# Attention loop written out group by group: three sets of load buffers, attention outputs three groups behind, x stored from SyncE's queue

## The chip, the cores and the metric

The kernel runs on one core of one Trainium2 chip. The metric is the device time of one execution in microseconds (us), lower is better. The core has five engines that work side by side: TensorE (PE: matrix products, its weight loads are listed as PEld), VectorE (DVE), ScalarE (ACT), GpSimd (POOL) and SyncE (SP, which here only issues transfers). DMA transfers are issued from SP's queue, ACT's queue or POOL's queue and are moved by 16 DMA engines that all of them share.

## The reference

Attention over 32 learned memory slots, then a dense layer with a gate, then a mixture of eight experts:

```python
a = exp(phi - max(phi, axis=2)); a = a / (sum(a, axis=2) + 1e-9)      # 8 x 8 heads, 576 x 32
k_m, v_m = a^T k, a^T v                                               # 32 x 64 per head
s = q k_m^T / 8; attn = exp(s - max(s)); attn = attn / (sum + 1e-9)   # 576 x 32 per head
x = attn v_m                            # all heads: 4608 tokens x 512
h = x @ w_in                            # 4608 x 2048
x2 = (h * sigmoid(1.702 * h)) @ w_out   # 4608 x 512
e = argmax(x2 @ w_gate)                 # one of 8 experts for each token
out = gate * sigmoid(x2 @ w_output_gate)[e] * (relu(x2 @ w1[e]) @ w2[e])
```

## The kernel before

The program has three stages. Stage A is the attention, in 16 groups of four heads (NG = 16; batch b is groups 2b and 2b+1). Stage B is the dense layer and the routing, in nine tiles of 512 tokens. Stage C is the experts, in blocks of 128 tokens. The change touches stage A and the first tile of stage B.

**A group of stage A.** SP loads `phi` (288 KB), `k` and `v` in one piece `kvm` (1152 KB) and `q` (576 KB) into one of two sets of buffers. DVE takes the maximum of phi (`phi_in`, L1147), ACT the exponential (L880), PE transposes it (L627, L630), ACT copies it out (`a_out`, L890), PE forms k_m and v_m (L647, L652), ACT scales them (`kv_scale`, L899), POOL lays v out in blocks (`v_blocks`, L1571), PE transposes k (L662), ACT copies it (`k_out`, L906), and PE makes the scores (L675). DVE transposes the scores and subtracts their maximum (`less_max`, L1158 to L1162), ACT takes the exponential (`exp_scores`, L884), DVE forms the inverse sums (`inverses`, L1169 to L1175), POOL multiplies (`normalize`, L1563), DVE transposes the result into `pT` (`attn_out`, L1181), PE multiplies it with v in two halves (`out_half`, L619), and ACT copies each half (`x_out`, L915) into `keep`, where x stays in on-chip memory (`xo` for the last batch).

**The order of the work** is written by hand. Each engine runs one program, and what it does for group g is mixed with work for the groups behind: in PE's `group(g)` stand the k/v products of g, the transposes of phi of g+1, the k transposes of g, the first half of the output of g-2, the scores of g, and the second half of the output of g-2. DVE's `group(g)` is `phi_in(g+1)`, `inverses(g)`, `less_max(g-1)`, `attn_out(g-2)`. There is one `pT`, which DVE fills and PE reads. Groups 0 to 2 and the last ones are written out, the others are a hardware loop of four groups a pass (`groups`, L376).

**SP's queue.** SP issues transfers in program order, and each waits until the buffer is free: `load_phi(g)` for exp of g-2 (L440), the k/v load for the k/v product of g-2, the q load for the scores of g-2. Between them it loads four quarters of `w_in` into the two halves of `raw`, which POOL splits into a high and a low part (`split_w_in`, L1548 and L1550; `split_w`, L1538 and L1540, for `w_out`). Each `load_w(n)` waits until part n-2 has been split.

**Into stage B.** ACT makes the high part of tile 0's x (`first_x_hi`, L941) in group 15, all four pieces. After group 15 it issues the store of batches 0 to 5 to DRAM from its own queue (`store_kept`, L921; 2 x 3456 KB), then batch 6 (2 x 576 KB), and later batch 7 (`store_last`, L927; 1152 KB). Tiles 1 and on load their x back from there. PE starts stage B with `mm1(0, 0)` (L702, 12 products of 128x512), `mm1(0, 1)` and `mm1(0, 2)` with the outputs of groups 14 and 15 between them; then `mm2(0, 0)`, `mm2(0, 1)` (L734), `mm1(0, 3)`, `mm2(0, 2)`, `mm1(0, 4)` and so on. `mm1(0, 4)` needs 12 split parts of weights, `mm2(0, f)` needs 5 + 2f: four parts are split in stage A, so for `mm1(0, 4)` POOL has to split parts 4 to 11 after it.

Of the kernel before, what the change touches and what calls it, by code (L numbers as in the profile page):

```python
# [91 lines left out]
def build(nc, q, kv, phi, w_in, w_out, gates, w1, w2, cst, out):  # L92
# [11 lines left out]
    with ExitStack() as ctx:  # L104
# [32 lines left out]
        with ExitStack() as a:  # L137


            vbd = sbt(a, "vbd", [P, 4, 2 * D])  # L140
            sc = [sbt(a, f"sc{u}", [P, S]) for u in range(2)]
            scs = sbt(a, "scs", [P, 2, 3, SB + 2])
            sbt(a, "before_xs", [P, K1 * T - 2 * S - 6 * (SB + 2)])

            qT, kvm, phT = [], [], []
            for u in range(2):
                qT.append(sbt(a, f"qT{u}", [P, QA // 2, HG, M]))
                kvm.append(sbt(a, f"kvm{u}", [P, QA * D * 2]))
# [8 lines left out]
            sbt(a, "before_aT", [P, S])  # L157
            aT = sbt(a, "aT", [P, S])
            am = sbt(a, "am", [P, S])
            sbt(a, "before_kmT", [P, QA * D])  # L160
            kmT = sbt(a, "kmT", [P, P])
            mask = sbt(a, "mask", [P, 2 * D])
            kvs = sbt(a, "kvs", [P, 2 * D])
            sbt(a, "before_pT", [P, S])
            pT = sbt(a, "pT", [P, S])
            xo = sbt(a, "xo", [P, 2, 2, S])
# [67 lines left out]
        s_phi = [sem(f"phi_loaded{u}") for u in range(2)]  # L234
        s_q = [sem(f"q_loaded{u}") for u in range(2)]
        s_kvl = [sem(f"kv_loaded{u}") for u in range(2)]
# [87 lines left out]

        def kept_at(b, u):

            return KEEP + u * KEPT * S + b * S
# [5 lines left out]
        def kept_stored(eng):  # L333

            eng.wait_ge(s_xfirst, 16 * 2)
            eng.wait_ge(s_xkept, 16 * 2)

        stage = [xo[:, 0, 0, 0:P], xo[:, 0, 0, P:2 * P]]
# [36 lines left out]

        def groups(eng, body):  # L376

            for g in range(3):
                body(g, g // 2, g)
            with eng.Fori(0, (NG - 4) // 4) as m:  # L380
                for j in range(4):
                    body(4 * m + (3 + j), 2 * m + (3 + j) // 2, (3 + j) % 4)
            body(NG - 1, B - 1, 3)
# [49 lines left out]
        def _(sp):  # L433
# [5 lines left out]
            def load_phi(g, b, u):  # L439

                wait(sp, s_aT, g - 1)
                sp.dma_start(phT[u][:], phi[bass.ds(g * P, P), :]).then_inc(s_phi[u], 16)

            def load_qkv(g, b, u):
# [5 lines left out]
                sp.dma_start(qT[u][:].rearrange("p c h n -> p (c h n)"), q[bass.ds(g * P, P), :]).then_inc(s_q[u], 16)  # L450
# [10 lines left out]
            load_phi(0, 0, 0)  # L461
# [3 lines left out]
            load_qkv(0, 0, 0)  # L465
            load_phi(1, 0, 1)
            load_qkv(1, 0, 1)
            def sp_group(g, b, r):

                u = r % 2  # L470
                if not isinstance(g, int) or g + 2 < NG:
                    load_phi(g + 2, b + 1, u)
                    load_qkv(g + 2, b + 1, u)

                if isinstance(g, int) and 1 <= g < 3:
                    load_w(g - 1, w_in_part(g - 1, 0))
                if isinstance(g, int) and g >= NG - 5 and g < NG - 3:
                    load_w(g - (NG - 5) + 2, w_in_part(g - (NG - 5) + 2, 0))


            for g in range(3):
                sp_group(g, g // 2, g)
            with sp.Fori(0, (NG - 8) // 4) as m:
                for j in range(4):
                    sp_group(4 * m + (3 + j), 2 * m + (3 + j) // 2, (3 + j) % 4)
            for g in range(NG - 5, NG - 2):
                sp_group(g, g // 2, g % 4)

# [18 lines left out]
            def sp_tile(t, first=False, last=False):  # L507
# [3 lines left out]
                if first:  # L511
                    for k in range(1, 4):
# [5 lines left out]
                        if k == 1:  # L518
                            sp.wait_ge(s_xfirst, 16 * 2)
                            sp.wait_ge(s_pT, NG)  # L520
                            load_x(t + 1)
# [81 lines left out]
        def _(pe):  # L603
            def out_half(g, r, i, bank=None):
# [3 lines left out]
                if i == 0:  # L608
                    wait(pe, s_pT, g + 1)
                    wait(pe, s_vbd, g + 1)  # L610


                if isinstance(g, int) and g >= NG - 2:
                    pe.wait_ge(s_xo, 2 * (NG - 2) + (1 if g == NG - 1 else 0))
                else:
                    wait(pe, s_xo, 2 * g - 1 + i)
                for pair in range(2):
                    rows = slice(pair * 64, pair * 64 + 64)
                    mm = pe.matmul(ps[:, bank + pair, 0:HS], vbd[rows, r, :], pT[rows, i * HS:(i + 1) * HS],  # L619
# [14 lines left out]
            def group(g, b, r):  # L634

                u = r % 2
                has_out = not isinstance(g, int) or g >= 2
                last = isinstance(g, int) and g == NG - 1

                wait(pe, s_kvl[u], 16 * (b + 1))  # L640
                if not isinstance(g, int) or g >= 3:
                    wait(pe, s_xo, 2 * g - 5)
                hold(pe, s_am, g + 1)
# [12 lines left out]
                if not last:  # L656
# [3 lines left out]
                hold(pe, s_kk, g + 1)  # L660
# [5 lines left out]
                if has_out:  # L666
                    out_half(g - 2, (r + 2) % 4, 0)

                wait(pe, s_kmT, g + 1)
                wait(pe, s_q[u], 16 * (b + 1))  # L670
                hold(pe, s_dv, DVE_A * g)
# [7 lines left out]
                if has_out:  # L679
                    out_half(g - 2, (r + 2) % 4, 1)  # L680

            wait(pe, s_cst, 2 * 16)
            a_transposes(0)
            groups(pe, group)
# [22 lines left out]

            mm1(0, 0)
            for i in range(2):
                out_half(NG - 2, (NG - 2) % 4, i, (4, 2)[i])  # L710
            mm1(0, 1)
            for i in range(2):
                out_half(NG - 1, (NG - 1) % 4, i, (6, 4)[i])
# [160 lines left out]
        def _(act):  # L874
            def exp_phi(g, u):
# [4 lines left out]
                act.activation(aT[:], phT[u][:], ACT.Exp, bias=amax[:, u, 0:1], accum_out=scs[:, u, 1, SB:SB + 1]).then_inc(s_aT, 1)  # L880
# [27 lines left out]
            def x_out(g, b, u, i, bank=None):  # L908
                bank = (4, 2)[i] if bank is None else bank
                hold(act, s_o, 2 * g + i + 1)  # L910
                if isinstance(b, int) and b == KEPT:
                    to = xo[:, u, :, i * HS:(i + 1) * HS]
                else:
                    to = keep_v[:, :, bass.ds(kept_at(b, u) + i * HS, HS)]
                act.copy(to, ps[:, bank:bank + 2, 0:HS]).then_inc(s_xo, 1)  # L915

            def store_kept(b, n, stored):

                act.wait_ge(s_xo, 4 * (b + n))
                for u in range(2):  # L920
                    act.dma_start(xT_dram[2 * u * P:(2 * u + 2) * P, b * S:(b + n) * S].rearrange("(a p) n -> p a n", a=2),  # L921
                                  keep_v[:, :, kept_at(b, u):kept_at(b + n, u)]).then_inc(stored, 16)
# [14 lines left out]
            def first_x_hi(c):  # L937

                act.wait_ge(s_sc, NG - 1)
# [3 lines left out]
            def group(g, b, r):  # L943
                u = r % 2
                last = isinstance(g, int) and g == NG - 1
                if not last:
                    exp_phi(g + 1, 1 - u)
                if not isinstance(g, int) or g >= 3:
                    x_out(g - 3, b - 2 + u, 1 - u, 1)
# [4 lines left out]
                if not isinstance(g, int) or g:  # L954
                    exp_scores(g - 1, 1 - u)
                k_out(g)
                if not last:
                    a_out(g + 1)
                else:
                    store_kept(0, KEPT - 1, s_xfirst)  # L960
                if not isinstance(g, int) or g >= 2:
                    x_out(g - 2, b - 1, u, 0)
# [118 lines left out]
            x_out(NG - 1, B - 1, 1, 0, 6)  # L1081
            x_out(NG - 1, B - 1, 1, 1, 4)
# [60 lines left out]
        def _(dve):  # L1143
            def phi_in(g, b, u):
                wait(dve, s_phi[u], 16 * (b + 1))

                dve.tensor_reduce(amax[:, u, 0:1], phT[u][:], AX.X, ALU.max, negate=True).then_inc(s_amax, 1)  # L1147
# [29 lines left out]
            def attn_out(g, u):  # L1177
# [11 lines left out]
            def group(g, b, r):  # L1189
# [536 lines left out]
```

## Time and profile before

| | |
|---|---|
| median of 3 runs | 1368.81 us (1366.98 to 1371.24) |
| profiled execution, its own time | 1368.63 us |
| its span in the trace | 1367.0 us |
| granted TensorE clock, mean | 0.987 of full speed |
| PE busy | 1317.9 us (96%), 6866 instructions |
| DVE busy | 635.1 us (46%) |
| ACT busy | 390.8 us (29%) |
| POOL busy | 549.2 us (40%) |
| chain that ended last | PE 85%, DMA 3% of the span |

The chain is followed back from the last instruction: at each step to what released it. Busy time is an average over the stages, so a change in one stage is read from that stage's part of the trace. "PEclk" is the clock that was granted to TensorE as a share of full speed (2.4 GHz; 0.50 is 1.2 GHz). "DMA share" is the mean busy share of the 16 DMA engines.

### The profile page before, as it was taken

Reading aid. Unit: us, or ns where it says so; the run is one execution under the profiler, and the core shown is the slowest. Engines: PE = TensorE matmul, PEld = TensorE weight load, DVE = VectorE, ACT = ScalarE, POOL = GpSimd, SP = SyncE. Lnnn points to the kernel's source line nnn. Section 1 sums busy time; section 2 is a strip of 40 time slices with the busy share of each in tenths; the row PEclk is TensorE's granted clock in tenths of the full one; section 3 lists DMA queues with packets and bytes.
Section 4 is the critical chain, followed back from the end, with each engine's and each line's share of the span. In section 5 each row is a group of like instructions: output and inputs, shape, how many; then the busy total and the mean of one; then the engine's idle time right before and its main releaser. Section 6 shows DMA issues by size and latency. Waiting matters only on the chain.

```text
span 1367.0 us, 23811 instructions
## 1 busy us (share of the span) xinstructions
PE 1317.9 (96%) x6866; PEld 1056.9 (77%) x6867; DVE 635.1 (46%) x1291; ACT 390.8 (29%) x725; POOL 549.2 (40%) x648
## 2 busy tenths in 40 slices
PE   5888899999999999999999999999999999999997
PEld 3445688888888888888888888887788888888886
DVE  4776243353343433534334344346655555555553
ACT  3564122222222222322222222223332222232221
POOL 2335683353454433443444334511533343433332
PEclk9899999999999999999999999999999999999999
DMA  8897437556566465465654646547884789648882
GB/s 316 319 352 304 156 130 210 192 184 183 189 213 179 169 192 190 151 189 177 180 187 163 192 172 173 177 159 261 228 229 101 202 228 268 177 118 254 251 245 63
DMA packets 152376, 274.19 MB, mean 201 GB/s; under 512 B 16916, under 2 KB 54053, under 8 KB 149765
## 3 DMA queue, kind: packets, MB, share of 16 engines
q1 hardware_dynamic: 94468, 196.04, 43.2%
q10 hardware_dynamic: 44672, 45.63, 13.2%
q0 software_dynamic: 13184, 31.88, 7.5%
q8 instruction: 27, 0.44, 0.1%
q14 instruction: 25, 0.20, 0.0%
HBM read 144.98 MB, written 100.45 MB: 180 GB/s over the span
## 4 chain that ended last, share of the span: by engine, by line
PE 85%; DMA 3%; POOL 1%; issue 1%; DVE 1%; ACT 0%; ACTq 0%; POOLq 0%
PE ps L702 28%; PE ps L734 28%; PE ps L804 14%; PE ps L775 14%; DMA raw<-in_moe_w_in 2%; PE ps L744 1%; DMA cq<-ch 1%; DMA cmeta<-record_scratch 0%; POOL W L1550 0%; ACTq L1036 0%; DVE chT L1371 0%; POOL W L1548 0%; DVE cqT L1358 0%; POOL out L1663 0%; POOL W L1540 0%
## 5 line engine op out<-in xcount | busy, mean ns | idle before, releaser
L702 PE MATMUL ps<-xs,W 128*128 (+1 forms) x1728 | 419.2, 391 | 3.0 <-POOL W L1550 3.0
L734 PE MATMUL ps<-W,gs 128*128 128x512 f32 x1728 | 417.0, 390 | 4.3 <-POOL W L1540 4.2
L734 PEld LDWEIGHTS ps<-W,gs 128*128 128x128 f32 x1728 | 325.2, 188 | 73.1 <-issue 5.0
L702 PEld LDWEIGHTS ps<-xs,W 128*128 128x128 f32 x1728 | 324.0, 188 | 73.3 <-issue 6.5
L1234 DVE TENSOR_TENSOR gate<-ps,gate 128x512 f32<-128x512 f32 x144 | 99.6, 692 | 373.0 <-ACT gate L978 370.4
L978 ACT ACTIVATE gate<-ps 128x512 f32<-128x512 f32 x144 | 86.2, 598 | 477.6 <-PE ps L702 453.4
L804 PE MATMUL ps<-W,chT 128*128 (+1 forms) x936 | 218.4, 389 | 2.5 <-DVE chT L1371 2.5
L775 PE MATMUL ps<-W,cx 128*128 (+1 forms) x936 | 218.6, 389 | 0.8 <-issue 0.8
L1604 POOL CAST whi<-raw 128x512 fp32r<-128x512 f32 x128 | 82.9, 648 | 331.4 <-DMA raw<-in_moe_w 331.4
L804 PEld LDWEIGHTS ps<-W,chT 128*128 128x128 f32 x936 | 175.5, 188 | 39.9 <-issue 3.6
L775 PEld LDWEIGHTS ps<-W,cx 128*128 128x128 f32 x936 | 175.5, 188 | 37.8 <-issue 1.4
L1606 POOL TENSOR_TENSOR raw<-raw,whi 128x512 f32<-128x512 f32 x128 | 171.5, 1340 | 21.5 <-POOL whi L1604 19.1
L1236 DVE TENSOR_TENSOR gs<-gate,gs 128x512 fp32r<-128x512 f32 x144 | 118.5, 823 | 99.9 <-ACT gs L982 99.2
L364 POOL DMA_DIRECT2D crec<-record_scratch x160 | 90.4, 565 | 184.5 <-DMA out<-cy,cmeta 120.2
L982 ACT CAST gs<-gate 128x512 fp32r<-128x512 f32 x144 | 89.4, 621 | 112.1 <-DVE gate L1234 109.5
L1043 ACT CAST chT<-cqT 128x512 fp32r<-128x512 f32 x41 | 25.4, 621 | 202.6 <-issue 159.8
L1663 POOL DMA_INDIRECT out<-cy,cmeta x39 | 44.1, 1132 | 78.4 <-ACT cy L1051 71.0
L1612 POOL DMA_INDIRECT record_scratch<-rec,posi x36 | 36.2, 1006 | 90.4 <-DVE posi L1300 81.8
L1371 DVE TENSOR_TENSOR chT<-cqT,chT 128x512 fp32r<-128x512 f32 x78 | 53.2, 691 | 39.2 <-ACT chT L1043 37.6
L1335 DVE TENSOR_TENSOR cx<-cxT,cx 128x512 fp32r<-128x512 f32 x40 | 43.7, 1091 | 56.7 <-ACT cx L1011 54.3
L1349 DVE TENSOR_SCALAR ch<-ps 128x512 f32<-128x512 f32 x37 | 25.5, 690 | 68.6 <-PE ps L775 68.3
L1358 DVE STREAM_TRANSPOSE cqT<-cq 128x512 f32<-128x512 f32 x78 | 50.6, 687 | 13.3 <-DMA cq<-ch 10.7
(163 smaller groups left out, 786.1 us busy)
## 6 DMA issues: line engine op xcount, KB each, us to landing
W<-expert_scratch SPq DMA_DIRECT2D x24, 2048.0 KB, 11.2
raw<-in_moe_w SPq DMA_DIRECT2D x128, 256.0 KB, 2.8
expert_scratch<-whi SPq DMA_DIRECT2D x128, 256.0 KB, 2.6
expert_scratch<-raw SPq DMA_DIRECT2D x128, 256.0 KB, 2.9
cq<-ch ACTq DMA_DIRECT2D x156, 128.0 KB
kvm<-in_kv SPq DMA_DIRECT2D x16, 1152.0 KB, 7.3
crec<-record_scratch POOLq DMA_DIRECT2D x160, 64.0 KB
qT<-in_q SPq DMA_DIRECT2D x16, 576.0 KB, 5.1
```

The costliest lines, as they stand in the source:

```text
L364: eng.dma_start(crec[b * M:(b + 1) * M, r % 3], rows[:, b * P:(b + 1) * P].rearrange("(h n) d -> n h d", n=M)).then_inc(loaded, 16)
L702: mm = pe.matmul(ps[:, f % 2, :], W[:, col:col + P], xs[:, bass.ds(x0 + (x_lo * K1 + c) * T, T)], start=(c == 0 and w_lo + x_lo == 0), sto ...
L734: mm = pe.matmul(ps[:, 2 + s, :], gs[:, f % 2, g_lo, s * P:(s + 1) * P], w_out_sb[:, f, w_lo, :], start=(f == 0 and g_lo + w_lo == 0), sto ...
L775: mm = pe.matmul(ps[:, 3 * u + j, :], cx[:, u, x_lo, c, :], W[:, bass.ds(col, 512)], start=(c == 0 and x_lo + w_lo == 0), stop=(c == K1 - ...
L804: mm = pe.matmul(ps[:, 5 + r % 2, :], chT[:, r % 2, h_lo, c, :], W[:, bass.ds(col, DM)], start=(c == 0 and h_lo + w_lo == 0), stop=(c == C ...
L978: act.activation(gate[:, f % 2, :], ps[:, f % 2, :], ACT.Sigmoid, scale=QTOK).then_inc(b_sig, 1)
L982: act.copy(gs[:, f % 2, 0, :], gate[:, f % 2, :]).then_inc(b_ghi, 1)
L1234: dve.tensor_tensor(gate[:, f % 2, :], ps[:, f % 2, :], gate[:, f % 2, :], ALU.mult).then_inc(b_g, 1)
L1236: dve.tensor_tensor(gs[:, f % 2, 1, :], gate[:, f % 2, :], gs[:, f % 2, 0, :].bitcast(F32), ALU.subtract).then_inc(b_glo, 1)
L1371: dve.tensor_tensor(by_h(1, j), cqT[:, j * 512:(j + 1) * 512].rearrange("p (h c n) -> p h c n", h=2, n=M), by_h(0, j).bitcast(F32), ALU.su ...
L1604: pool.tensor_copy(whi[:, u, :], raw[:, u, :]).then_inc(e_hi, 1)
L1606: pool.tensor_tensor(raw[:, u, :], raw[:, u, :], whi[:, u, :].bitcast(F32), ALU.subtract).then_inc(e_lo, 1)
```

## The change

1. **Load buffers.** There are three sets in place of two (`qT2`, `kvm2`, `phT2` are new), taken in turn by g % 3. `load_phi(g)`, `load_kv(g)` and `load_q(g)` wait for exp, k/v product and scores of group g-3 in place of g-2.
2. **Outputs.** `out_half` for group g-3 stands where that of g-2 stood, and there are two `pT`, taken in turn. `x_out` follows one group later. More of the outputs therefore falls behind group 15: a pair of halves is now ahead of, and one behind, `mm1(0, 0)`.
3. **Unrolled.** `groups` is gone; all 16 groups are written out on every engine.
4. **Weights.** The four quarters of `w_in` are loaded and split at groups 5, 6, 9, 10 in place of 1, 2, 11, 12 on SP (2, 3, 12, 13 on POOL).
5. **x of tile 0.** `first_x_hi` is made two pieces in group 14 and two in group 15.
6. **Stores.** Batches 0 to 4 are stored in one go (2 x 2880 KB), 5 and 6 one by one, and from SP's queue, in program order ahead of `load_w(6)`. Batch 7 stays on ACT's queue.

Core of the diff:

```diff
-        s_phi = [sem(f"phi_loaded{u}") for u in range(2)]
+        s_phi = [sem(f"phi_loaded{u}") for u in range(3)]
...
+        FIRST = 5
+        QUARTER = (5, 6, 9, 10)
...
-            def load_phi(g, b, u):
-                wait(sp, s_aT, g - 1)
+            def load_phi(g):
+                wait(sp, s_aT, g - 2)
...
-                wait(sp, s_kv, g - 1)
-                sp.dma_start(kvm[u][:], kv[bass.ds(g * P, P), :]).then_inc(s_kvl[u], 16)
-                wait(sp, s_sc, g - 1)
+            def load_kv(g):
+                wait(sp, s_kv, g - 2)
+                sp.dma_start(kvm[g % 3][:], kv[g * P:(g + 1) * P, :]).then_inc(s_kvl[g % 3], 16)
+            def load_q(g):
+                wait(sp, s_sc, g - 2)
...
+            for g in range(1, NG):
+                load_phi(g)
+                load_kv(g)
+                load_q(g)
+                if g in QUARTER:
+                    c = QUARTER.index(g)
+                    load_w(c, w_in_part(c, 0))
             load_w(K1, w_out_v[0])
             load_w(K1 + 1, w_in_part(0, 1))
+            store_kept(0, FIRST, s_xfirst)
+            for b in range(FIRST, KEPT):
+                store_kept(b, 1, s_xkept)
...
-                if has_out:
-                    out_half(g - 2, (r + 2) % 4, 0)
+                if g >= 3:
+                    out_half(g - 3, 0)
...
+            out_half(NG - 3, 0)
             mm1(0, 0)
-            for i in range(2):
-                out_half(NG - 2, (NG - 2) % 4, i, (4, 2)[i])
+            out_half(NG - 3, 1)
+            out_half(NG - 2, 0)
             mm1(0, 1)
+            out_half(NG - 2, 1)
             for i in range(2):
-                out_half(NG - 1, (NG - 1) % 4, i, (6, 4)[i])
+                out_half(NG - 1, i, (6, 4)[i])
             mm1(0, 2)
...
-                if last:
-                    for c in range(K1):
-                        first_x_hi(c)
+                if g >= NG - 2:
+                    for c in range(2):
+                        first_x_hi(2 * (g - (NG - 2)) + c)
...
-                wait(dve, s_o, 2 * g)
-                dve.transpose(pT[:], sc[u][:]).then_inc(s_pT, 1)
+                wait(dve, s_o, 2 * (g - 1))
+                dve.transpose(pT[g % 2][:], sc[g % 2][:]).then_inc(s_pT, 1)
```

How it moves two pieces of the program. First SP, from the loads of group 15 to the first parts of weights of stage B (`raw` holds a part of weights, `xT_scratch` is x in DRAM). Before:

```order
L442 DMA phT<-in_phi 128x576
L447 DMA kvm<-in_kv 128x2304
L450 DMA qT<-in_q 128x1152
L455 DMA raw<-in_moe_w_out 128x512
L455 DMA raw<-in_moe_w_in 128x512
L455 DMA raw<-in_moe_w_out 128x512
L455 DMA raw<-in_moe_w_in 128x512
```

and with the change:

```order
L442 DMA phT<-in_phi 128x576
L447 DMA kvm<-in_kv 128x2304
L452 DMA qT<-in_q 128x1152
L464 DMA raw<-in_moe_w_out 128x512
L464 DMA raw<-in_moe_w_in 128x512
L458 DMA xT_scratch<-keep 128x2x2880 x2
L458 DMA xT_scratch<-keep 128x2x576 x4
L464 DMA raw<-in_moe_w_out 128x512
L464 DMA raw<-in_moe_w_in 128x512
```

The six stores now stand between parts 4 and 5 and parts 6 and 7.

Second PE, from the k/v products of group 15 to `mm2(0, 0)` (`pT` with `vbd` is an output, `xs` with `W` is `mm1`, `W` with `gs` is `mm2`). Before:

```order
L647 MATMUL ps<-kvm,am 32x128 x16
L652 MATMUL ps<-kvm,am 32x128 x4
L662 MATMUL ps<-ident,kvs 64x128 x2
L619 MATMUL ps<-pT,vbd 128x288 x2
L675 MATMUL ps<-qT,kmT 32x288 x8
L619 MATMUL ps<-pT,vbd 128x288 x2
L702 MATMUL ps<-xs,W 128x512 x12
L619 MATMUL ps<-pT,vbd 128x288 x4
L702 MATMUL ps<-xs,W 128x512 x12
L619 MATMUL ps<-pT,vbd 128x288 x4
L702 MATMUL ps<-xs,W 128x512 x12
L734 MATMUL ps<-W,gs 128x512 x24
```

and with the change:

```order
L643 MATMUL ps<-kvm,am 32x128 x16
L648 MATMUL ps<-kvm,am 32x128 x4
L658 MATMUL ps<-ident,kvs 64x128 x2
L618 MATMUL ps<-pT,vbd 128x288 x2
L671 MATMUL ps<-qT,kmT 32x288 x8
L618 MATMUL ps<-pT,vbd 128x288 x4
L699 MATMUL ps<-xs,W 128x512 x12
L618 MATMUL ps<-pT,vbd 128x288 x4
L699 MATMUL ps<-xs,W 128x512 x12
L618 MATMUL ps<-pT,vbd 128x288 x6
L699 MATMUL ps<-xs,W 128x512 x12
L733 MATMUL ps<-W,gs 128x512 x24
```

Two output halves more (four products) stand behind group 15's own work: one ahead of `mm1(0, 0)` and one ahead of `mm1(0, 2)`, and the outputs beside group 15's scores belong to group 12 in place of 13.

## Rows read from the trace of the kernel before

**Rows 1.** Chain that ended last, first 200 us: start us, us, what.

```profile
121.78 12.74 DMA raw<-in_moe_w_in
...
148.64 4.34 PE ps L702 x12
152.97 2.72 PE ps L734 x12
```

**Rows 2.** Windows: us, busy us (instructions) per engine, granted clock, DMA share, GB/s.

```profile
12.00:18.00 6.00, 3.08 (x32) 1.65 (x36) 0.98 (x3) 1.59 (x5) 0.45 (x1) 1.00 1.02 425
20.00:104.00 84.00, 69.41 (x992) 36.30 (x988) 60.56 (x113) 46.76 (x100) 28.37 (x33) 0.88 0.93 336
69.00:69.50 0.50, 0.50 (x7) 0.12 (x5) 0.19 (x1) 0.50 (x2) 0.00 (x0) 1.00 0.82 166
70.00:70.50 0.50, 0.50 (x12) 0.30 (x4) 0.50 (x2) 0.50 (x2) 0.00 (x0) 1.00 0.98 406
76.71:82.20 5.49, 4.67 (x79) 2.57 (x77) 4.50 (x9) 3.70 (x9) 2.13 (x2) 1.00 0.98 342
106.00:114.00 8.00, 4.17 (x71) 2.28 (x72) 7.11 (x13) 5.82 (x12) 4.35 (x5) 1.00 0.05 18
115.00:140.00 25.00, 21.85 (x108) 15.26 (x92) 11.32 (x17) 8.85 (x14) 11.33 (x13) 0.95 1.00 409
```

**Rows 3.** Waits, 0 to 120 us: us in total, times, longest us.

```profile
DVE csum L1147 <- DMA phT<-in_phi: 27.7, 16, 3.7
...
PE ps L619 <- DVE pT L1181: 15.2, 10, 2.1
```

**Rows 4.** DVE in order of time: start us, us, what [idle before <-releaser].

```profile
18.34 0.75 DVE L1147 TENSOR_REDUCE csum<-phT 128x1 f32<-128x576 f32 x1 [3.70 <-DMA phT<-in_phi]
...
23.98 0.75 DVE L1147 TENSOR_REDUCE csum<-phT 128x1 f32<-128x576 f32 x1 [2.30 <-DMA phT<-in_phi]
...
75.06 0.75 DVE L1147 TENSOR_REDUCE csum<-phT 128x1 f32<-128x576 f32 x1 [0.49 <-DMA phT<-in_phi]
...
80.93 0.75 DVE L1147 TENSOR_REDUCE csum<-phT 128x1 f32<-128x576 f32 x1 [0.88 <-DMA phT<-in_phi]
...
102.89 0.75 DVE L1147 TENSOR_REDUCE csum<-phT 128x1 f32<-128x576 f32 x1 [3.24 <-DMA phT<-in_phi]
```

**Rows 5.** PE in order of time, 20 to 165 us.

```profile
28.93 1.33 PE L619 MATMUL ps<-pT,vbd 64*128 64x288 f32 x4 [1.96 <-DVE pT L1181]
...
81.51 0.76 PE L619 MATMUL ps<-pT,vbd 64*128 64x288 f32 x4
...
117.02 3.20 PE L702 MATMUL ps<-xs,W 128*128 128x512 f32 x12
...
148.64 4.34 PE L702 MATMUL ps<-xs,W 128*128 128x512 f32 x12 [2.99 <-POOL W L1550]
```

**Rows 6.** SP, ACT and POOL in order of time, seven places.

```profile
67.84 0.33 SPq L447 DMA_DIRECT2D kvm<-in_kv  x1
...
110.69 2.18 ACT L941 CAST xs<-keep 128x512 fp32r<-128x512 f32 x4
...
113.76 0.98 ACTq L921 DMA_DIRECT2D xT_scratch<-keep  x2
...
119.87 0.33 SPq L455 DMA_DIRECT2D raw<-in_moe_w_out  x1
...
130.62 0.61 POOL L1538 CAST W<-raw 128x512 fp32r<-128x512 f32 x1 [8.86 <-DMA raw<-in_moe_w_out]
...
156.42 0.61 POOL L1538 CAST W<-raw 128x512 fp32r<-128x512 f32 x1 [0.86 <-DMA raw<-in_moe_w_out]
...
161.13 0.61 POOL L1538 CAST W<-raw 128x512 fp32r<-128x512 f32 x1 [0.81 <-DMA raw<-in_moe_w_out]
```

**Rows 7.** DMA issues, 0 to 130 us: KB each, median us to landing.

```profile
kvm<-in_kv SPq DMA_DIRECT2D x16, 1152.0 KB, 7.3
...
phT<-in_phi SPq DMA_DIRECT2D x16, 288.0 KB, 5.2
```

More of the change, by code:

```diff
@@ L374, in wait_records @@
                 wait(eng, c_rec[r], 80 * (i // RING if r == EARLY else i // RING + 1))
[L376 to L383, printed above, removed]
         def tiles(eng, tile):
@@ L603, in _, with out_half @@
         def _(pe):
-            def out_half(g, r, i, bank=None):
+            def out_half(g, i, bank=None):
                 bank = (4, 2)[i] if bank is None else bank
                 if i == 0:
[L609 to L614, printed above, removed]
+                    pe.wait_ge(s_pT, g + 1)
+                    pe.wait_ge(s_vbd, g + 1)
+                if g == NG - 1:
+                    pe.wait_ge(s_xo, 2 * (NG - 2) + 1 + i)
                 else:
@@ L632, in a_transposes, with group @@
                 tr.then_inc(s_atr, 1)
[L634 to L643, printed above, removed]
+            def group(g):
+                u = g % 3
+                pe.wait_ge(s_kvl[u], 16 * (g // 3 + 1))
+                wait(pe, s_xo, 2 * (g - 4) + 1)
+                pe.wait_ge(s_am, g + 1)
                 out_of = lambda h: ps[h * M:(h + 1) * M, 4, 3 * P:4 * P].rearrange("p (w d) -> p w d", w=2)
@@ L654, in group @@
                 mm.then_inc(s_kv, 1)
-                if not last:
+                if g + 1 < NG:
                     a_transposes(g + 1)
                 wait(pe, s_kmT, g)
-                hold(pe, s_kk, g + 1)
+                pe.wait_ge(s_kk, g + 1)
                 for i in range(2):
@@ L677, in group @@
                 mm.then_inc(s_sc, 1)
-                if has_out:
-                    out_half(g - 2, (r + 2) % 4, 1)
-            wait(pe, s_cst, 2 * 16)
+                if g >= 3:
+                    out_half(g - 3, 1)
+            pe.wait_ge(s_cst, 2 * 16)
             a_transposes(0)
-            groups(pe, group)
+            for g in range(NG):
+                group(g)
             def mm1(t, f):
@@ L1187, in x_lo, with group @@
                                   ALU.subtract).then_inc(b_xlo, 1)
-            def group(g, b, r):
-                u = r % 2
-                last = isinstance(g, int) and g == NG - 1
-                two = not isinstance(g, int) or g >= 2
-                if not last:
-                    phi_in(g + 1, b + u, 1 - u)
-                inverses(g, u, two, True)
-                if not isinstance(g, int) or g:
+            def group(g):
+                u = g % 2
+                if g + 1 < NG:
+                    phi_in(g + 1)
+                inverses(g, u, g >= 2, True)
+                if g:
                     less_max(g - 1, 1 - u)
-                if two:
-                    attn_out(g - 2, u)
+                if g >= 2:
+                    attn_out(g - 2)
             dve.memset(padrec[:], 0.0).then_inc(b_setup, 1)
@@ L1216, in _ @@
             dve.wait_ge(s_cst, 2 * 16)
-            groups(dve, group)
+            for g in range(NG):
+                group(g)
             dve.wait_ge(b_xhi, K1)
```

171 lines of the change are left out of this document (78 added, 93 removed).

## The prediction

> **What bounds the kernel now.** I read the page's chain first: PE is 85% of it, and DMA, its second part, lies in its first 150 us. [Rows 1] show where: the chain waits 12.74 us for one 256 KB part of weights at 121.78 us and reaches `mm1(0, 4)` on PE at 148.64; from there on it is PE without a break. So whatever brings `mm1(0, 4)` forward shortens the kernel by as much, and nothing else in this change does. I then split the 148.64 us into three stretches. G14 is the instant at which DVE takes the maximum of phi of group 15 (102.89 us, [rows 4]); T is the start of `mm1(0, 0)` (117.02 us, [rows 5]); the third ends at `mm1(0, 4)`.
>
> *First stretch.* DVE waited 27.7 us in all 16 groups for phi to land ([rows 3]), and phi is what it begins a group with. Between two such waits a group takes it 80.93 - 0.88 - 75.06 = 4.99 us ([rows 4]), while the groups came (102.89 - 23.98) / 12 = 6.58 us apart. PE's own work in a group is 4.67 us at full clock ([rows 2], fifth line). So loads set the pace. But not by bandwidth alone: in 20 to 104 us the DMA engines are busy 0.93 of the time and yet move 336 GB/s, while in 12 to 18 us, when SP had issued several loads ahead, they moved 425 GB/s at full share ([rows 2]). The difference stands at the start of a load that was issued late: SP issues k/v at 67.84 us ([rows 6]), and the share stays at 0.82 while only 166 GB/s move at 69.0 to 69.5; a microsecond later it is 406 ([rows 2]). With two sets of buffers each group has such starts.
>
> *Second stretch.* 14.1 us from G14 to T. *Third stretch.* 148.64 - 117.02 = 31.6 us. The DMA engines stand idle from 106 to 114 us (share 0.05) and are then full from 115 to 140 us at 409 GB/s ([rows 2]), since ACT issues the stores only at 113.76 ([rows 6]). Part 6 of the weights is issued at 119.87, and POOL gets it at 130.62 ([rows 6]), 10.7 us for 256 KB.
>
> **The change, part by part.** Times are against the profiled execution, 1368.63 us; the median is 0.2 us above it.
>
> *Three load sets.* A group is 1152 + 576 + 288 KB = 2.06 MB ([rows 7]; q is half of k/v): 4.86 us at 425 GB/s, 5.72 us at the rate 336 / 0.93 = 361 GB/s that the busy engines had. Group 2's phi came at 18.34 us, as it will. Group 3's k/v wait is gone, so 2.06 MB later its phi is there at about 23.1 us in place of 23.98. From there 12 groups to G14. Floor by DVE: 12 x 4.99 = 59.9 us. Floor by DMA at 425 GB/s: 12 x 4.86 + 2.5 for four quarters of weights = 60.8 us. Upper bound, should late starts go but the rate stay at 361: 12 x 5.72 + 3 = 71.6 us. DVE, DMA and PE then lie within 0.3 us of each other, and they wait for each other; I take 5.3 us a group, nearer to the floors since the queue will be as deep as in 12 to 18 us, and 1.5 us for one stretch at half clock early on, as at 28.93 us, where 0.76 becomes 1.33 ([rows 5]). G14 = 23.1 + 63.6 + 1.5 = 88.2 us: **-14.7 us** (bounds -19 and -8).
>
> *Outputs three behind, two pT.* PE waited 15.2 us for `pT` ([rows 3]). As DVE set the pace, that wait was cover and costs nothing now; once loads are fed it would be on the path (scores stand behind it on PE), so this edit has no term of its own: it is what permits 5.3 in place of about 6. The same holds for the register instructions of the loop. If the cover were gone without this edit, each group would lose up to 2.1 us, the longest such wait.
>
> *G14 to T.* ACT's four casts (2.18 us, [rows 6]) stood ahead of group 15's k/v scaling; two of them move to group 14, where ACT has slack (3.70 of 5.49 us busy, [rows 2]). Against it, one more output half (0.76 us) precedes `mm1(0, 0)`. I take **-1.5 us** (bounds 0 and -2.2).
>
> *T to `mm1(0, 4)`.* PE's own work between them is four `mm1` and three `mm2` of 2.72 us each ([rows 1], third line), 19.0 us, five output halves of about 0.7 us, and one wait of about 1 us for ACT, which now computes the gate ahead of two output copies: about T + 24. The weights: POOL needs (161.13 - 156.42) = 4.71 us for a pair of parts ([rows 6]), so from the landing of part 6 to the twelfth split are three pairs less a gap, 9.4 + 3.9 = 13.4 us. When does part 6 land? It now stands behind all stores on SP's queue. All loads with parts 4 and 5 end at about 18 + 30.1 MB / 0.42 = 90 us at the earliest; then 2 x 2880 KB and 2 x 576 KB, 7.1 MB at 409 GB/s, 17.3 us; then batch 6, 2.9 us, and the part, 0.6, and some 1.5 us to be seen: 112.5 us, T + 11.7 with T = 100.8. That gives `mm1(0, 4)` at T + 25.2; batch 7, issued from ACT's queue near T + 9, takes a share, so I say T + 25.5: **-6.1 us** (bounds -7.6, PE alone, and -2).
>
> What the edit does to the queue must be counted against it: SP now waits for the copy of group 13's second half before it may issue part 6, about T + 5 in place of T + 2.9. It is hidden, because the stores ahead in the queue end later than that. A rule of the Trainium skill speaks against the move: "DMA: Bandwidth & Descriptors", queues, rings and completion order, says in substance that each DMA engine takes turns between the queue rows that have work, while one row is served in order. By it, part 6 on a row of its own would not wait out batch 6 and the part would come about 2 us earlier, so the third term would be -7.6 in place of -6.1. The trace of before does not separate the two, as there the part took 10.7 us even on its own row.
>
> *Clock.* `mm1(0, 4)` took 4.34 us after its waits, the next step 2.72 ([rows 1]); without the wait ahead it keeps full clock: **-1.6 us** (bounds 0 and -1.6).
>
> Weights at groups 5, 6, 9, 10: POOL has 2.13 of 5.49 us busy in a group ([rows 2]), a split takes 1.9; hidden. If not, `normalize` is late and DVE's `pT` with it.
>
> Sum: -14.7 - 1.5 - 6.1 - 1.6 = -23.9 us, 1368.6 - 23.9 = **1344.7 us**.
>
> A faster stage A does not add much: the landing of part 6 at 112.5 us is set by bytes alone. With G14 at 83.5 `mm1(0, 4)` could not start before 112.5 + 13.4 = 125.9 us, 22.7 earlier than before, plus 1.6: 1344.3 us. Only a rate above 409 to 425 GB/s goes below, some 440 for 40 MB giving 4 us more: 1340.
>
> **Rivals.**
> (a) *The rate does not recover.* The loads stay at 361 GB/s with a full queue. For it: the share is already 0.93. Against: 12 to 18 us. G14 = 23.1 + 71.6 = 94.7, -8.2; the loads end near 100 us, the stores 17 us later, part 6 near 122.5 with T = 107.3, so `mm1(0, 4)` at T + 28.6, -3.0. With -1.5 and -1.6: 1354.3 us.
> (b) *The buffers do not do what they are for.* SP issues in order, and q of group g, which waits for scores, stands ahead of phi of g+1; if that keeps the queue short, G14 stays and only -1.5, -6.1 and -1.6 are left: 1359.4 us. Against: scores of g-3 are a whole group older than what was waited for.
> (c) *PE falls to half clock and becomes the bound; slower.* A group of 4.67 us becomes 4.67 x 1.33 / 0.76 = 8.2 us, as in the rows at 28.93 and 81.51 ([rows 5]). If it stays there, 12 x 8.2 = 98 us, G14 = 121.5, +18.6; with -6.1 and the tail as before, 1381 us. It decides from (102.9 + 9.2 - 23.1) / 12 = 7.4 us a group. For it: the granted clock was 0.88 in 20 to 104 us ([rows 2]), and PE's group is now on the path. Against: it fell after idle time of about 2 us, as that of 1.96 us before 28.93 ([rows 5]), and these waits are what goes. The Trainium skill, "TensorE: Matmul & The Clock Gate", the part on the clock gate, says that activity releases the lower clock and idleness restores it; the trace agrees in that row.
>
> **How the numbers follow.** The forecast's mechanism, stage A near 5.3 us a group and the stores under its end, 0.60; (a) 0.22; (b) 0.10; (c) 0.04; something between no change and (b), 0.04. A measurement tells 0.3% (4.1 us) from no change. The forecast alone spans 1340 to 1350 us; to hold (a) and most of what is between it and (b) the range goes up to 1358 us. Every case but (c) and part of the last is faster by over 4.1 us: faster 0.94, same 0.02, slower 0.04.
>
> **What would show it.** Right: waits of DVE for phi after group 3 under 5 us in sum (18 before); groups 5.0 to 5.5 us apart; G14 at 85 to 91 us; 390 to 425 GB/s while the queue is full; no idle DMA between loads and stores; `mm1(0, 4)` at 123 to 129 us at full clock. Wrong: phi waits that stay with the share at 1 (a) or with gaps (b); a granted clock below 0.8 in stage A (c); part 6 landing later than T + 14, which would make the stores on SP's queue the new wait.

## Result, and the profile after

| | before | changed |
|---|---|---|
| median, us (4 runs each) | 1370.03 | 1348.22 |
| lowest to highest, us | 1366.98 to 1373.23 | 1344.54 to 1349.71 |
| profiled execution, us | 1368.63 | 1348.39 |
| its span, us | 1367.0 | 1346.8 |

The ratio is 0.9837 with a 95% interval of 0.9805 to 0.9868: faster by 1.6%, 3.5 us above the forecast of 1344.7 and inside its range. The profiled executions differ by 20.24 us. By the terms of the prediction, measured between the same instants of the two traces:

| | forecast, us | measured, us | from |
|---|---|---|---|
| first stretch, to G14 | -14.7 | -16.2 | 102.89 to 86.68 |
| G14 to T | -1.5 | -1.7 | 14.13 to 12.42 |
| T to `mm1(0, 4)` | -6.1 | -1.5 | 31.62 to 30.07 |
| duration of `mm1(0, 4)` | -1.6 | +1.1 | 4.34 to 5.46 |
| behind it | 0 | -1.9 | the rest of 20.24 |
| sum | -23.9 | -20.2 | |

The total is near in part by luck: the third and fourth terms missed by 7.3 us, and 3.6 us came back elsewhere, 1.9 of it at a place where the forecast had nothing. First the stretch that came out better. Windows of the changed kernel (columns as in [rows 2]):

```profile
12.00:18.00 6.00, 2.65 (x24) 1.50 (x20) 1.08 (x5) 1.12 (x3) 0.45 (x1) 1.00 1.02 423
20.00:80.00 60.00, 53.99 (x861) 30.06 (x854) 53.10 (x102) 38.56 (x86) 27.59 (x30) 0.94 1.01 410
20.00:86.70 66.70, 60.46 (x952) 33.62 (x944) 59.63 (x114) 43.13 (x97) 30.79 (x33) 0.95 1.02 412
102.00:108.00 6.00, 5.47 (x29) 3.46 (x28) 5.12 (x8) 4.68 (x8) 2.80 (x3) 1.00 1.01 400
```

12 to 18 us is as it was. Behind it the rate of 423 GB/s now nearly holds: 412 to the end of stage A where [rows 2] had 336, at a share of 1.02 where it was 0.93. DVE is now busy 59.6 of 66.7 us, near full. The granted clock rose from 0.88 to 0.95, so PE did not fall to half clock for good, as rival (c) had it. It fell twice for a short while, to 0.50, at 30 to 32 us and at 46 to 48 us, after PE had waited 1.98 and 1.41 us for ACT; DVE's groups there were 4.88 and 4.89 us apart all the same, so no cost shows there. DVE's maxima of phi, changed kernel, groups 5 to 8 and 15 (columns as in [rows 4]):

```profile
33.78 0.75 DVE L1139 TENSOR_REDUCE csum<-phT 128x1 f32<-128x576 f32 x1
...
40.05 0.75 DVE L1139 TENSOR_REDUCE csum<-phT 128x1 f32<-128x576 f32 x1 [1.37 <-DMA phT<-in_phi]
...
45.56 0.75 DVE L1139 TENSOR_REDUCE csum<-phT 128x1 f32<-128x576 f32 x1 [0.62 <-DMA phT<-in_phi]
...
50.45 0.75 DVE L1139 TENSOR_REDUCE csum<-phT 128x1 f32<-128x576 f32 x1
...
86.68 0.75 DVE L1139 TENSOR_REDUCE csum<-phT 128x1 f32<-128x576 f32 x1
```

Phi of group 3 came at 23.98 us, as before. From there to 86.68 are 62.7 us for 12 groups, 5.23 us each where it was 6.58. Only four of them waited for phi (the two here and 1.16 and 0.62 us at 61.66 and 67.18 us), 3.8 us in all where 5 was forecast at most. They are groups 6, 7, 10 and 11, each one behind a group in which a part of the weights is loaded: these four took 5.8 us on average, the other eight 4.93, about DVE's own time for a group (4.99, [rows 4]).

Then the stretch that did not. The chain of waits of the changed kernel (columns as in [rows 1]), and below it SP and POOL in order of time (columns as in [rows 6]):

```profile
105.17 8.36 DMA raw<-in_moe_w_out
...
117.95 2.95 DMA raw<-in_moe_w_in
...
122.98 4.04 DMA raw<-in_moe_w_in
...
129.17 5.46 PE ps L699 x12
134.63 2.85 PE ps L733 x12
```

```profile
84.44 20.68 SPq L458 DMA_DIRECT2D xT_scratch<-keep  x6
105.17 0.51 SPq L464 DMA_DIRECT2D raw<-in_moe_w_out  x1
...
102.90 0.61 POOL L1539 CAST W<-raw 128x512 fp32r<-128x512 f32 x1
...
113.58 0.61 POOL L1529 CAST W<-raw 128x512 fp32r<-128x512 f32 x1 [8.70 <-DMA raw<-in_moe_w_out]
...
118.39 0.61 POOL L1529 CAST W<-raw 128x512 fp32r<-128x512 f32 x1 [0.46 <-DMA raw<-in_moe_w_out]
120.96 0.61 POOL L1539 CAST W<-raw 128x512 fp32r<-128x512 f32 x1 [0.60 <-DMA raw<-in_moe_w_in]
...
127.08 0.61 POOL L1539 CAST W<-raw 128x512 fp32r<-128x512 f32 x1 [1.57 <-DMA raw<-in_moe_w_in]
```

The six stores occupy SP's queue up to 105.12 us, each waiting there for its copies; part 6 leaves at 105.17 and POOL has it at 113.58, behind what the stores have still to move. So the wait of 8.86 us for this part in [rows 6] is there again, 8.70 us, only 17 us earlier. That is T + 14.5, just past the T + 14 that the forecast named as the sign that the stores had become the new wait (a second execution, e5 below, has T + 13.5). The same chain then runs through two more parts (117.95, 122.98), which the forecast had counted as POOL's time alone. The first of these is not late for bytes. The DMA engines are busy a third of the time by then (columns as in [rows 2]):

```profile
116.00:120.00 4.00, 4.00 (x19) 3.32 (x18) 0.09 (x1) 0.00 (x0) 3.38 (x4) 1.00 0.35 117
```

`raw` has two halves, so each part is issued only when the part two before it has been split. Part 9 is issued at 117.95 us, as the split of part 7 ends (117.93), and POOL begins with it at 120.96, 3.0 us later; part 11 is issued at 122.98, as the split of part 9 ends (122.95), and is begun at 127.08, 4.1 us later, with the load of x of tile 1 (1024 KB, issued at 123.44) beside it. PE, around its last wait (columns as in [rows 5]), and a window on it:

```profile
99.10 3.01 PE L699 MATMUL ps<-xs,W 128*128 128x512 f32 x12
...
129.17 5.46 PE L699 MATMUL ps<-xs,W 128*128 128x512 f32 x12 [5.06 <-POOL W L1541]
134.43 3.05 PE L733 MATMUL ps<-W,gs 128*128 128x512 f32 x12
```

```profile
129.20:134.40 5.20, 5.20 (x12) 4.07 (x13) 0.00 (x0) 0.00 (x0) 3.16 (x4) 0.50 0.27 88
```

PE idles longer for the same split than before, 5.06 us where [rows 5] had 2.99, and does the next twelve products at a granted clock of 0.50, 1.2 GHz, in nearly twice the time (5.46 us; the steps behind it take 2.88).

### The profile page after: what moved, and what is told of

It is laid out like the page before. It is cut to its first block, busy times and chain, and to the rows that moved or that the text cites. A ratio compares the mean times of both kernels' runs of the same rounds, so it can differ in the third digit from the quotient of the medians.

```text
span 1346.8 us, 23538 instructions
## 1 busy us (share of the span) xinstructions
PE 1309.3 (97%) x6866; PEld 1054.9 (78%) x6867; DVE 634.2 (47%) x1291; ACT 388.6 (29%) x725; POOL 554.6 (41%) x648
## 4 chain that ended last, share of the span: by engine, by line
PE 90%; DMA 4%; DVE 2%; issue 1%; POOL 1%; SPq 1%; ACT 0%; ACTq 0%; POOLq 0%
PE ps L699 29%; PE ps L733 28%; PE ps L774 15%; PE ps L803 15%; DMA phT<-in_phi 3%; PE ps L743 1%; DMA raw<-in_moe_w_out 1%; DMA raw<-in_moe_w_in 1%; DVE sc L1150 0%; DVE scs L1152 0%; DVE scs L1161 0%; PE ps L618 0%; PE ps L671 0%; POOL W L1541 0%; DMA cq<-ch 0%
```

## Experiments

All times are medians, each with its ratio to the kernel before on the same chip. G14, T and `mm1(0, 4)` are read in each trace as above.

**e1, the unrolling alone.** The kernel before, with the groups of all engines written out:

```diff
-            for g in range(3):
-                body(g, g // 2, g)
-            with eng.Fori(0, (NG - 4) // 4) as m:
...
-            body(NG - 1, B - 1, 3)
+            for g in range(NG):
+                body(g, g // 2, g % 4)
```

> The kernel before, with the 16 groups written out on every engine and nothing else changed. Theory (loads and stores set the pace, the loop's own instructions lie under the waits for phi): within 0.3% of before, G14 (DVE's maximum of phi of group 15) at 101 to 104 us, mm1(0, 4) at 147 to 150 us. Rival (the loop's register work and branches cost on the path): some 0.5 us a group, 5 to 8 us faster.

1369.82 us, ratio 1.0006 (0.9988 to 1.0024). G14 103.34, waits for phi 30.0 us, `mm1(0, 4)` at 150.62. The unrolling, with the register instructions that go with it, brings nothing that a measurement can tell.

**e2, three sets of buffers, but loads that wait as with two.**

```diff
-                wait(sp, s_aT, g - 2)
+                wait(sp, s_aT, g - 1)
...
-                wait(sp, s_kv, g - 2)
+                wait(sp, s_kv, g - 1)
...
-                wait(sp, s_sc, g - 2)
+                wait(sp, s_sc, g - 1)
```

> The changed kernel, but loads wait for exp, k/v product and scores of group g-2 as with two sets. Theory (the late starts of loads cost the 16 us of stage A): waits for phi come back to 15 to 20 us after group 3, the rate in 20 to 80 us falls to 330 to 370 GB/s from 410, G14 moves from 86.7 us to 98 to 103 us. As the stores then end later too, mm1(0, 4) moves by less or as much: 8 to 16 us slower than the changed kernel. Rival (outputs three behind and two pT brought the gain): G14 at 87 to 92 us, under 4 us slower.

1364.23 us, ratio 0.9959 (0.9940 to 0.9979). Waits for phi and the windows, e2:

```profile
DVE csum L1139 <- DMA phT<-in_phi: 26.7, 14, 3.8
```

```profile
20.00:80.00 60.00, 48.03 (x720) 26.36 (x712) 43.99 (x84) 31.28 (x71) 22.46 (x26) 0.91 0.95 340
```

The phi waits are back and the rate has fallen back to 340 GB/s, with the share at 0.95: the DMA engines look busy and move a sixth less. G14 is 100.56 and `mm1(0, 4)` starts at 146.50. So the third set, by how early it lets a load be issued, is worth 16 us of the 22, and all else in the change together some 6 (3 to 8 by the interval). Outputs, weights, x of tile 0 and the place of the stores are not separated in these 6, other than by e3 for the outputs.

**e3, outputs two groups behind as before, all else as changed.** Small edits on PE and ACT, of which the main ones:

```diff
-                if g >= 3:
-                    out_half(g - 3, 0)
+                if g >= 2:
+                    out_half(g - 2, 0)
...
-                if g >= 4:
-                    x_out(g - 4, 1)
+                if g >= 3:
+                    x_out(g - 3, 1)
```

> The changed kernel with three load sets and two pT, but outputs of g-2 beside group g as before. Theory (with loads fed, PE's wait for pT is on the path, since scores stand behind it): groups 5.8 to 6.6 us apart in place of 5.2, G14 at 93 to 103 us, but the stores then start with it, so the whole is 5 to 14 us slower than the changed kernel. Rival (that wait stays covered): groups stay at 5.2 us, G14 below 89 us, within 3 us of the changed kernel.

1347.50 us, ratio 0.9841 (0.9817 to 0.9866): no slower than the changed kernel, so I was wrong. Windows and the waits for `pT`, e3:

```profile
20.00:80.00 60.00, 53.08 (x848) 29.20 (x844) 53.20 (x99) 39.92 (x86) 26.81 (x30) 0.97 1.02 420
```

```profile
PE ps L618 <- DVE pT L1169: 7.4, 8, 1.5
```

PE still waits 7.4 us for `pT`, and it costs nothing, since DVE and the loads set the pace (G14 86.29). Outputs three groups behind are worth nothing here; e8 beside e6, and e9 beside e10, will say the same.

**e5, the changed kernel again**, unedited, beside the runs below.

> The changed kernel once more, on the same chip as the three below, to compare them with. 1344 to 1351 us, part 6 of the weights at POOL at 112 to 115 us, mm1(0, 4) at 127 to 130 us and at half clock after its wait.

1347.73 us, ratio 0.9839 (0.9818 to 0.9860). G14 85.37, T 97.80, part 6 at POOL 111.30, `mm1(0, 4)` at 127.53 after 5.58 us of idle time, 5.46 us long. The wait and the half clock at `mm1(0, 4)` are there again. What differs is stage A: 420 GB/s in 20 to 80 us where the first trace had 410, at a granted clock of 1.00, and part 6 at T + 13.5.

**e4, the stores issued from ACT's queue.**

```diff
+            def store_kept(b, n, stored):
+
+                act.wait_ge(s_xo, 4 * (b + n))
+                for u in range(2):
+                    act.dma_start(...
...
+                if g == 2 * FIRST + 3:
+                    store_kept(0, FIRST, s_xfirst)
+                if g == NG - 1:
+                    store_kept(FIRST, 1, s_xkept)
```

> The changed kernel with the same stores at the same points of x, but issued by ACT on its own queue. Part 6 of the weights then shares the DMA engines with the stores in place of standing behind them. Theory (taking turns lets it through): it is issued at about 103 us and lands at 106 to 109 us in place of 113.6, mm1(0, 4) at 123 to 127 us at full clock in place of 129.2, 3 to 7 us faster than the changed kernel. Rival: ACT is held up while it issues the 5.9 MB store beside a full queue, its copies come late and G14 moves back by 3 to 8 us, no gain or a loss; or loads of groups 14 and 15 are slowed by the turns, with the same effect.

1347.87 us, ratio 0.9833 (0.9809 to 0.9857): no difference, where I had expected 3 to 7 us. POOL in order of time, five of the parts 5 to 11, then ACT and PE, e4:

```profile
105.03 0.61 POOL L1540 CAST W<-raw 128x512 fp32r<-128x512 f32 x1 [2.44 <-DMA raw<-in_moe_w_in]
109.18 0.61 POOL L1530 CAST W<-raw 128x512 fp32r<-128x512 f32 x1 [1.77 <-DMA raw<-in_moe_w_out]
112.91 0.61 POOL L1540 CAST W<-raw 128x512 fp32r<-128x512 f32 x1 [1.77 <-DMA raw<-in_moe_w_in]
...
119.76 0.61 POOL L1540 CAST W<-raw 128x512 fp32r<-128x512 f32 x1 [2.94 <-DMA raw<-in_moe_w_in]
...
125.91 1.16 POOL L1540 CAST W<-raw 128x512 fp32r<-128x512 f32 x1 [2.24 <-DMA raw<-in_moe_w_in]
```

```profile
95.50 1.14 ACT L930 CAST xs<-keep 128x512 fp32r<-128x512 f32 x2 [1.81 <-issue]
```

```profile
97.04 0.44 PE L647 MATMUL ps<-ident,kvs 128*64 128x128 f32 x4 [2.68 <-ACT kvs L887]
...
101.48 3.01 PE L688 MATMUL ps<-xs,W 128*128 128x512 f32 x12
...
128.56 4.47 PE L688 MATMUL ps<-xs,W 128*128 128x512 f32 x12 [2.23 <-POOL W L1542]
```

Part 6 does come earlier, by 4.4 us against the first trace of the changed kernel and 2.1 us against e5 (issued 102.61, at POOL 109.18), so the stores let it through. But parts 7, 9 and 11 are then late by 1.8 to 2.9 us, and T itself comes at 101.48, 2.4 us later than in the first trace, though G14 is the same (86.46). That delay is ACT's: it issues the store of batch 5 at 93.72 us, which takes 1.68 us, and stands idle for 1.81 us over it, ahead of the k/v scaling of group 15. PE waits 2.68 us for that scaling (0.77 in the changed kernel) and then does the last steps ahead of T in part at half clock (granted clock 0.58 from 97 to 101 us). My rival had ACT held up in this way, though ahead of G14 and not behind it. So this run does not tell what a queue row of its own would be worth if another engine than ACT issued the stores.

The prediction weighed a rule of the Trainium skill here ("DMA: Bandwidth & Descriptors", queues, rings and completion order), by which a queue row of its own would bring the part forward. This trace agrees as to the part. The third stretch is shorter too, 27.1 us where the changed kernel has 30.1 and 29.7 in its two traces, and ACT's delay ahead of T has taken that back.

**e6, the last two stores behind the parts.** The store of batch 5 goes behind parts 6 and 7, that of batch 6 behind 8 and 9.

```diff
-            for b in range(FIRST, KEPT):
-                store_kept(b, 1, s_xkept)
...
+                            if f in (1, 2):
+                                store_kept(FIRST + f - 1, 1, s_xkept)
```

> The changed kernel, but batch 5 is stored behind parts 6 and 7 of the weights, batch 6 behind parts 8 and 9. The large store of batches 0 to 4 stays. Theory (part 6 stands behind the bytes of these stores, and the later parts do not need the DMA engines all the time): part 6 at POOL at 106 to 109 us in place of 113.6, mm1(0, 4) at 122 to 126 us at full clock (2.7 us in place of 5.5), 4 to 8 us faster than the changed kernel. Rival (the bytes only change places: every 256 KB part now waits behind one 1.2 MB store or the store of batch 7): part 6 early, but parts 8 to 11 late, mm1(0, 4) at 127 to 130 us as before, within 1.5 us of the changed kernel.

1344.80 us, ratio 0.9809 (0.9783 to 0.9835). Part 6 at POOL 108.66 (T + 8.8), `mm1(0, 4)` 126.70 (T + 26.8) after 3.21 us of waiting, 4.58 us long. POOL now waits 3.56 us for part 8, which stands behind the store. I had expected `mm1(0, 4)` at full clock and 4 to 8 us; it is still at half clock for part of the step. Where the changed kernel had 400 GB/s, e6 has

```profile
102.00:108.00 6.00, 6.00 (x32) 3.85 (x31) 5.46 (x8) 4.07 (x6) 3.57 (x3) 1.00 0.74 267
```

as SP issues part 7, with the store behind it, only when its buffer is free (105.68 us). At `mm1(0, 5)` e6's PE is 1.9 us ahead of e5's: a gain, though less than half of the 4.7 us by which POOL's wait for part 6 fell (7.71 in e5, 3.00 in e6). The intervals of e5 and e6 overlap, so the times of this run alone do not settle it; e8, which moves the same two stores, has the same ratio.

**e7, the same, two parts later still** (batch 5 behind parts 8 and 9, batch 6 behind 10 and 11).

```diff
-                            if f in (1, 2):
-                                store_kept(FIRST + f - 1, 1, s_xkept)
+                            if f in (2, 3):
+                                store_kept(FIRST + f - 2, 1, s_xkept)
```

(The edit is against e6.)

> As e6, but batch 5 is stored behind parts 8 and 9, and batch 6 behind parts 10 and 11. Theory: parts 6 to 9 are free of the stores of batches 5 and 6 and meet only that of batch 7 on ACT's queue, mm1(0, 4) at 121 to 125 us at full clock, as e6 or 1 us faster. Rival: part 12 may only be written once batches 0 to 6 are stored, and x of tile 1 stands behind batch 6; then POOL waits there and mm1(0, 8) or mm2(0, 4) is late, the gain of e6 is given back in part.

1346.82 us, ratio 0.9835 (0.9808 to 0.9862), within its error of the changed kernel. PE and ACT, e7:

```profile
124.20 3.00 PE L699 MATMUL ps<-xs,W 128*128 128x512 f32 x12 [1.23 <-POOL W L1541]
...
128.34 3.04 PE L733 MATMUL ps<-W,gs 128*128 128x512 f32 x12 [1.14 <-DVE gs L1227]
```

```profile
125.49 0.60 ACT L969 ACTIVATE gate<-ps 128x512 f32<-128x512 f32 x1 [9.97 <-DMA xT_scratch<-keep]
```

`mm1(0, 4)` comes at T + 24.8, at full clock, which is what the prediction had for the changed kernel. The price is elsewhere: ACT waits 9.97 us for the late store, so the gate and with it `mm2(0, 3)` are late, and POOL waits 5.38 us for part 12. `mm1(0, 8)` then waits 2.56 us for a split and takes 4.58 us, part of it at half clock. The wait moved behind the place the prediction looked at.

**e8, e3 and e6 together.**

```diff
-                    out_half(g - 3, 0)
+                    out_half(g - 2, 0)
...
+                            if f in (1, 2):
+                                store_kept(FIRST + f - 1, 1, s_xkept)
```

> e3 and e6 together: outputs two groups behind with two pT, three load sets, and batches 5 and 6 stored behind parts 6, 7 and 8, 9. With the outputs three behind worth nothing, it equals e6 within 2 us (3 to 8 us faster than the changed kernel). Rival: outputs three behind matter once the stores no longer set mm1(0, 4); then it is over 2 us slower than e6.

1343.41 us, ratio 0.9809 (0.9784 to 0.9834). T 97.36, `mm1(0, 4)` 123.74 after 3.83 us, again 5.46 us long. No further gain over e6 that a measurement can tell. Against e3, which has outputs two behind as well, `mm2(0, 3)` comes 3.4 us earlier (129.00 for 132.39), so the move of the two stores shows again, at 2 to 4 us by the traces and the medians.

**e9 and e10, eight parts split in stage A.** If bytes and splits behind T are the trouble, parts 6 and 7 belong ahead of it. Eight of the groups take one part each in place of four, POOL splits them among the groups too, and parts 8 and 9 follow the store of batches 0 to 4. Four splits are then left behind the stores in place of six. e9 has outputs two groups behind, e10 three.

```diff
-        QUARTER = (5, 6, 9, 10)
+        QUARTER = (4, 5, 7, 8, 10, 11, 13, 14)
...
-            load_w(K1, w_out_v[0])
-            load_w(K1 + 1, w_in_part(0, 1))
...
+            load_w(8, w_out_v[2])
+            load_w(9, w_in_part(2, 1))
```

> e3 (outputs two behind, three load sets) with eight parts of the weights loaded and split in stage A (groups 4, 5, 7, 8, 10, 11, 13, 14) in place of four; parts 8 and 9 stand right behind the store of batches 0 to 4 on SP's queue, the stores of batches 5 and 6 behind them. Theory (in the changed kernel mm1(0, 4) waits for the twelfth split, while POOL was idle half of stage A): stage A up to 2.5 us longer for 1 MB more, only four splits left behind it, mm1(0, 4) at 120 to 125 us without a wait and at full clock, 5 to 9 us faster than the changed kernel: 1339 to 1343 us. Rival (the DMA engines are full either way, so the bytes of the parts only come off the loads' time, and later parts stand behind the same stores): G14 back by 3 us or more, mm1(0, 4) or mm1(0, 8) waits all the same, within 3 us of the changed kernel.

> The changed kernel (outputs three behind) with the same eight parts in stage A and the same order of stores as e9. Theory: equals e9 within 2 us. Rival: with one more output pair behind group 15 it is over 2 us slower than e9.

1342.49 us, ratio 0.9807 (0.9787 to 0.9828), and 1343.02 us, ratio 0.9808 (0.9791 to 0.9825): the lowest two medians, 4 to 5 us below the changed kernel. They ran on another chip than e5 to e8, so the ratios are what compares: 0.9839 for e5, whose interval overlaps those of e9 and e10 by a little, and 0.9809 for e6 and e8, which the times cannot tell from these two. The traces say more: at `mm1(0, 5)` PE is 5.0 (e9) and 4.3 us (e10) ahead of e5, 3.1 and 2.5 us ahead of e6, 1.5 and 0.8 us ahead of e8. PE in order of time, e9:

```profile
102.68 3.65 PE L699 MATMUL ps<-xs,W 128*128 128x512 f32 x12
...
122.55 2.88 PE L731 MATMUL ps<-W,gs 128*128 128x512 f32 x12
125.27 2.88 PE L699 MATMUL ps<-xs,W 128*128 128x512 f32 x12
```

`mm1(0, 4)` no longer waits and keeps full clock. Stage A pays for it: G14 88.31 and 88.92 (85.37 in e5), T 102.68 and 101.18 (97.80). From T to `mm1(0, 4)` it takes 22.6 us in e9, below the T + 24 that I had as PE's own time. As both bytes and splits have moved ahead of T, these runs do not say which of the two it was; a third half of `raw`, which would separate them, was not run. What is left ahead of it is stage A, where DVE, DMA and PE are all near full.

## Why the prediction was right, and where it was not

1. *Loads set the pace of stage A, through late issue and not through bandwidth.* Right. 336 GB/s became 412 with the share up by 0.09 only, groups came 5.23 us apart, DVE waited 3.8 us for phi after group 3, and e2 took it back with nothing but the three waits. Forecast -14.7, measured -16.2: I had 5.3 us a group, and it was 5.23. I had 1.5 us for a stretch at half clock; there were two such stretches, and they cost DVE's groups nothing. e5 has none in 20 to 80 us, and its G14 is 1.3 us earlier, at a rate of 420 for 410 GB/s, so a small cost is not excluded. Against that, phi of group 3 came at 23.98 and not at 23.1. Rivals (a) and (b) are out: the rate rose, and only four groups waited.
2. *Rival (c), PE as the bound.* Out: granted clock 0.95 in stage A, and groups 5.23 us apart where (c) had 8.2. Its waits for `pT` went; those for ACT did not all go, and two of them brought the short stretches at half clock.
3. *"It is what permits 5.3 in place of about 6"*, of the outputs three behind. Wrong. e3 has two behind and G14 at 86.29. I took a wait of 15.2 us on PE for cover that would be uncovered. With loads fed and two `pT` it was 7.4 us on PE, and PE had the room for it, with 4.67 us of work in groups of 5.2. Whether the second `pT` is worth anything was not run by itself. The claim on register instructions in the same place held (e1).
4. *G14 to T.* Right, -1.7 for -1.5.
5. *T to `mm1(0, 4)`, -6.1.* This is the term that failed. It measured -1.5. Three things went into it. I had the queue's rate at 420 GB/s up to 90 us, and it was 410 (window 20 to 80), so what lies behind came later: part 6 at 113.58 for 112.5. In e5, where the rate was 420, it came at 111.30. T came 1.7 us earlier than forecast, which bytes do not follow. And from there to the twelfth split I counted 13.4 us, POOL's own time for three pairs; it took 15.6, as three of the next parts were themselves late (0.46, 0.60 and 1.57 us). For the most part that is not bytes but the two halves of `raw`: from issue to POOL these parts took 2.8, 3.0 and 4.1 us, at a DMA share of 0.35 from 116 to 120 us and 0.29 from 120 to 124, and none could be issued sooner. The forecast had no term for this. PE was therefore ready 5.06 us too soon.
6. *Clock, -1.6.* Failed with it: it rested on "without the wait ahead". With a wait of 5.06 us the step took 5.46, at half clock. e7 (1.23 us of waiting, 3.00 us long) and e9 (none, 2.88) show the term was sound where the wait does go. The Trainium skill, "TensorE: Matmul & The Clock Gate", the part on the clock gate, has idleness bring the lower clock back, and these rows agree.
7. *What the edit does to SP's queue.* I wrote that SP's wait for the copies of group 13 is hidden, since the stores ahead end later. SP issued part 6 at T + 6.1 and it was at POOL 8.4 us later. The DMA share was 1.00 to 1.01 from 100 to 108 us, over SP's wait and behind it, so it was hidden. In e4 SP has no such wait (part 6 issued at T + 1.1) and the kernel gains nothing, but the delay of ACT is in that time. That the order of stores and parts matters e6 and e8 show: 2 to 4 us for two stores moved.
8. *Behind `mm1(0, 4)`, 0.* The step after it is 18.3 us earlier, and PE's products keep that distance through stage B; 1.9 us more come at the passage from stage B to C. The prediction had said that nothing else in this change shortens the kernel. e1, in which neither loads nor stores differ from before, shows 1.8 us at the same place, so it need not come from the change. The most of it is one wait of PE for DVE's `chT` in the first block of stage C: 2.11 us in the trace of before, 0.79 in the changed kernel's, 0.71 in e1's, 0.70 in e5's. Why it is longer in that one execution stays open.

So the bound was read right and the size of the first gain too, while of the 7.7 us forecast for the third stretch and the clock 0.4 was left; PE stood idle or ran at half clock for the rest. In this trace, 1.5 us better at G14 did not reach `mm1(0, 4)`, as the prediction had said of a faster stage A. No run tests that by itself: in e5 G14 is 1.3 us earlier and `mm1(0, 4)` 1.6 us, but there the loads ran faster too.

## What to carry to other kernels

A DMA share of 0.93 did not mean here that the DMA engines were at their rate. In a kernel like this, compare the GB/s in a stretch in which the queue was deep with those of the rest, and if they differ, issue loads earlier (a third set of buffers) first. When a stage becomes faster, count the bytes that must land before the next stage can run, at the rate measured and not at the best one. Count the way from issue to use as well, wherever a transfer has to wait for one of two buffers. Put transfers that nobody waits for soon (here two stores) behind those that somebody does, though not so late that their buffer is missed. A wait that shows as large on an engine that isn't the bound may stay and cost nothing; removing it is not a gain until the trace with everything else in place says so.

## What the runs showed of the hardware beside that

- The loss from late issue is larger than the share tells: two sets gave 340 GB/s at a share of 0.95 (e2), three sets 410 to 420 at 1.01 to 1.02 (changed, e3).
- 256 KB on a queue row of its own, beside stores on another, took 6.6 us from issue to POOL (e4), where the same part behind the stores on one row took 8.4 (changed) and 7.6 us (e5), issued later.
- ACT stood idle for 1.81 us over the issue of two 576 KB stores from its own queue (e4, 93.72 us), and PE waited 2.68 us for what ACT did next.
- Idle time just ahead does not by itself say what clock the next step has: 2.23 us ahead of `mm1(0, 4)` left full clock in e2 (3.00 us) and not in e4 (4.47 us). The waits of 5.06, 5.20 and 5.58 us (changed, e3, e5) each cost 2.1 to 2.6 us in the step behind (4.95 to 5.46 us where 2.88 is full clock), and so did 3.83 us in e8 (5.46 us).
